# Hashed attention and two expert layers on one core: the first weight's sums spread over the loop, bucket marks by clipping, two reorderings

## What is computed

```python
# attention: 2 x 8 heads, 768 tokens, 64 wide
q_bits = (einsum('bhsd,dk->bhsk', q, proj) > 0)      # 6 hash bits a token
k_bits = (einsum('bhsd,dk->bhsk', k, proj) > 0)
mask = q_bucket[:, :, :, None] == k_bucket[:, :, None, :]
scores = where(mask, q @ k.T / sqrt(64), -1e9)
attn = softmax(scores); x = attn @ v                 # -> 1536 tokens x 512
# expert layer 1, dense: 8 experts, hidden 1024, 8 rounds of row and column scaling
P = exp(x @ w_gate - max); for _ in range(8): normalise rows, then columns of P
x = sum_e P[:, e] * (relu(x @ w1[e]) @ w2[e])
# expert layer 2, routed: each token with x @ w_skip > 0 goes to its best expert
x[t] += gate[t] * (relu(x[t] @ w1[e_t]) @ w2[e_t])
```

## Time and profile before

| what | value |
| --- | --- |
| median of 3 runs | 1365.22 us |
| the profiled execution's own time | 1366.09 us |
| its span, first to last instruction | 1364.3 us |
| PE busy | 1318.5 us (97%) |
| DVE busy | 850.2 us (62%) |
| ACT busy | 567.3 us (42%) |
| POOL busy | 332.9 us (24%) |
| mean granted TensorE clock | 0.993 of full speed |

### The profile page before, as it was taken

The page is one execution under the profiler, slowest core; times in us unless marked ns, Lnnn a source line. Parts: engine busy times, 40 slices in busy tenths (PEclk is TensorE's granted clock), DMA queues, the critical chain, the costliest instruction groups (busy, mean ns, idle before and its releaser), DMA issues.

```text
span 1364.3 us, 24719 instructions
## 1 busy us (share of the span) xinstructions
PE 1318.5 (97%) x9435; PEld 762.6 (56%) x9435; DVE 850.2 (62%) x1486; ACT 567.3 (42%) x870; POOL 332.9 (24%) x229
## 2 busy tenths in 40 slices
PE   6799999899999999999999999999999999998987
PEld 3576776655456446545545644554564465556665
DVE  5799999786667427525633743663474275567993
ACT  5799999653123204303411430431242043226662
POOL 4888889431100300300110030020003000121211
PEclk9899999999999999999999999999999999999999
DMA  8333532142011011001101100110110122467940
GB/s 227 97 93 92 127 93 49 63 166 98 0 63 62 1 62 61 0 0 61 61 0 61 61 0 0 62 61 0 61 61 0 36 83 82 167 208 271 340 166 21
DMA packets 51631, 109.84 MB, mean 81 GB/s; under 512 B 5216, under 2 KB 8840, under 8 KB 51568
## 3 DMA queue, kind: packets, MB, share of 16 engines
q1 hardware_dynamic: 48880, 105.40, 24.3%
q0 software_dynamic: 2240, 3.35, 0.7%
q10 hardware_dynamic: 448, 0.19, 0.1%
HBM read 93.57 MB, written 17.34 MB: 81 GB/s over the span
## 4 chain that ended last, share of the span: by engine, by line
PE 88%; DVE 4%; issue 2%; ACT 2%; DMA 0%; POOL 0%; ACTq 0%; POOLq 0%; DVEq 0%
PE ps L1676 14%; PE ps L1679 14%; PE ps L1680 14%; PE ps L1702 10%; PE ps L1705 10%; PE ps L1704 10%; PE ps L1597 5%; PE ps L1585 2%; PE ps L1587 2%; PE ps L1569 1%; PE ps L1607 1%; PE ps L1609 1%; PE ps L1611 1%; ACT probsT_hi L794 1%; DVE probsT_lo L1090 0%
## 5 line engine op out<-in xcount | busy, mean ns | idle before, releaser
L1702 PE MATMUL ps<-x_hi,w_hi 128*128 128x384 f16 x896 | 292.1, 326 | 3.2 <-DVE parts L1255 1.5
L1705 PE MATMUL ps<-x_hi,w_lo 128*128 128x384 f16 x896 | 292.1, 326 | 0.0
L1704 PE MATMUL ps<-x_lo,w_hi 128*128 128x384 f16 x896 | 292.1, 326 | 0.0
L1680 PE MATMUL ps<-w_hi,h 128*128 128x512 f16 x768 | 291.0, 379 | 0.0
L1679 PE MATMUL ps<-w_lo,h 128*128 128x512 f16 x768 | 291.0, 379 | 0.0
L1676 PE MATMUL ps<-w_hi,h 128*128 128x512 f16 x768 | 291.0, 379 | 0.0
L1312 DVE SCALAR_TENSOR_TENSOR x<-ps,gate_now,x 128x512 f32<-128x512 f32 x84 | 63.1, 751 | 251.7 <-PE ps L1680 250.7
L633 POOL TENSOR_TENSOR wf<-wf 128x1024 f32<-128x1024 f32 x8 | 18.8, 2353 | 632.7 <-PE ps L1705 622.1
L923 ACT ACTIVATE x1s<-ps 128x384 f32<-128x384 f32 x64 | 30.4, 475 | 327.0 <-PE ps L1705 327.0
L940 ACT ACTIVATE h<-parts 128x1152 f16<-128x1152 f32 x64 | 74.4, 1163 | 141.7 <-DVE parts L1270 141.7
L1680 PEld LDWEIGHTS ps<-w_hi,h 128*128 128x128 f16 x768 | 75.1, 98 | 90.6
(11 more groups left out here) (226 smaller groups left out, 2291.8 us busy)
## 6 DMA issues: line engine op xcount, KB each, us to landing
wf<-w1a SPq DMA_DIRECT2D x32, 512.0 KB, 6.0
w_stage_in<-w2a SPq DMA_DIRECT2D x8, 2048.0 KB, 8.8
w_in<-w1b SPq DMA_DIRECT2D x4, 2048.0 KB, 9.4
w_in<-w2b SPq DMA_DIRECT2D x4, 2048.0 KB
w_in_b<-w1b SPq DMA_DIRECT2D x4, 2048.0 KB, 10.6
w_in_b<-w2b SPq DMA_DIRECT2D x4, 2048.0 KB
rows<-blank SPq DMA_DIRECT2D x1, 6682.0 KB, 21.7
qk_in<-kT SPq DMA_DIRECT2D x32, 192.0 KB, 4.3
```

Of the source, the lines that this page charges most:

```text
L1680: last = pe.matmul(acc, a_lo, b_hi, start=False, stop=(m == n - 1))
L1702: pe.matmul(group_bank(g, role), w_hi, x_hi, start=(opens and kt == 0), stop=False, skip_group_check=not opens)
L1704: pe.matmul(group_bank(g, role), w_hi, x_lo, start=False, stop=False, skip_group_check=not opens)
L1705: last = pe.matmul(group_bank(g, role), w_lo, x_hi, start=False, stop=(kt == 1), skip_group_check=not opens)
```

## The change

It has four parts. (1) `sum_w1(0)` no longer stands ahead of POOL's round 1; its four sums come one each at the end of the rounds 1 to 4, and `split_first_w1` takes the blocks in an order in which each block's sum is there (5, 2, 0, 3, 1, 4, 6). (2) ACT takes the hash with the activation Identity, a scale of 2^112 and a per-partition bias, in place of Copy, and POOL clips it between `mark_floor` and `mark_top` by a minimum and a maximum, in place of a comparison and a product. DVE makes the bias from two small operations after the first head's marks; constants and the place of the negated projection follow. (3) In the last head ACT's `take_o` comes ahead of the work on x, and the high parts of x's blocks stand at the steps 1, 2, 4, 5 and after the last step, with none at step 3. (4) `split_gates` moves from group 1 to group 4 of the first expert.

```diff
+W1_SPLIT = (5, 2, 0, 3, 1, 4, 6)
...
-                pool.tensor_scalar(marks[HASHED, :], hashed[HASHED, :], least[HASHED, :], mark[HASHED, :],
-                                   ALU.is_ge, ALU.mult).then_inc(marks_ready, 1)
+                pool.tensor_scalar(marks[HASHED, :], hashed[HASHED, :], mark_top[HASHED, :], mark_floor[HASHED, :],
+                                   ALU.min, ALU.max).then_inc(marks_ready, 1)
...
+            def sum_w1_block(e, n):
+                if n == 0:
+                    pool.wait_ge(w1_loaded, 64 * e + 64)
+                    pool.tensor_tensor(wf[:, 5, :, :], wf[:, 0, :, :], wf[:, 3, :, :], ALU.subtract
+                                       ).then_inc(w1_summed, 1)
+                elif n == 1:
+                    pool.tensor_tensor(wf[:, 3, :, :], wf[:, 3, :, :], wf[:, 2, :, :], ALU.add
+                                       ).then_inc(w1_summed, 1)
+                elif n == 2:
+                    pool.wait_ge(w1_summed, 4 * e + 2)
+                    pool.tensor_tensor(wf[:, 4, :, :], wf[:, 3, :, :], wf[:, 0, :, :], ALU.subtract
+                                       ).then_inc(w1_summed, 1)
+                else:
+                    pool.wait_ge(w1_summed, 4 * e + 3)
+                    pool.tensor_tensor(wf[:, 6, :, :], wf[:, 1, :, :], wf[:, 4, :, :], ALU.subtract
+                                       ).then_inc(w1_summed, 1)
...
+            def split_first_w1(n):
+                k = W1_SPLIT[n]
+                pool.wait_ge(w1_summed, min(n + 1, 4))
...
-            sum_w1(0)
-            pool.wait_ge(w1_summed, 4)
             for j in range(1, G // 2):
...
                 normalise(2 * j - 1)
+                if j <= 4:
+                    sum_w1_block(0, j - 1)
                 split_first_w1(j - 1)
...
-                act.activation(hashed[HASHED, c * HALF:(c + 1) * HALF], psH[HASHED, 0:HALF], ACT.Copy
-                               ).then_inc(hash_taken, 1)
+                act.activation(hashed[HASHED, c * HALF:(c + 1) * HALF], psH[HASHED, 0:HALF], ACT.Identity,
+                               bias=hash_bias[HASHED, :], scale=HASH_SCALE).then_inc(hash_taken, 1)
...
                 if step in (0, 1):
                     take_xf(2 * step)
-                if step >= 1:
-                    x7_hi_part(0, X_HI[step - 1])
+                if step in (1, 2, 4, 5):
+                    x7_hi_part(0, X_HI[(1, 2, 4, 5).index(step)])
...
+                    if s % QT == 1 and not (first and s == 1):
+                        take_o(2 * j + s // QT - 1)
                     if last and s >= QT:
                         first_x(s - QT)
-                    if s % QT == 1 and not (first and s == 1):
-                        take_o(2 * j + s // QT - 1)
...
             act.wait_ge(zeroed, 12)
+            act.wait_ge(least_ready, 6)
             head_pairs(act, pair)
...
-            for k in X_HI[QT - 1:]:
+            for k in X_HI[QT - 2:]:
                 x7_hi_part(0, k)
...
             for c in range(2):
                 first_buckets(c)
+            dve.tensor_scalar(hash_bias[Q_MARKS, :], below_q[Q_MARKS, :], 0.5, Q_MASK, ALU.is_lt, ALU.mult
+                              ).then_inc(least_ready, 1)
+            dve.tensor_scalar(hash_bias[K_MARKS, :], below_k[K_MARKS, :], -K_MASK, None, ALU.mult
+                              ).then_inc(least_ready, 1)
...
-                    if first and g == 1:
+                    if first and g == 4:
                         split_gates()
```

More of the change, by code:

```diff
@@ L55 @@
 Q_MASK, K_MASK = 2.0 ** 15, 2.0 ** 13
-SMALLEST = 2.0 ** -126
+SMALLEST, HASH_SCALE = 2.0 ** -126, 2.0 ** 112
 MARKS = 2 * NBITS
@@ L118, in build @@
         least = sb("least", [P, 1], fp32)
-        mark = sb("mark", [P, 1], fp32)
+        hash_bias = sb("hash_bias", [P, 1], fp32)
+        mark_top = sb("mark_top", [P, 1], fp32)
+        mark_floor = sb("mark_floor", [P, 1], fp32)
         eps_bias = sb("eps_bias", [P, 1], fp32)
@@ L622, in _ @@
             split_k(1, 1)
-            pool.wait_ge(least_ready, 5)
+            pool.wait_ge(least_ready, 4)
             mark_buckets(1, 0, None)
@@ L646, in split_first_w1 @@
-            def split_first_w1(k):
+            def sum_w1_block(e, n):
[14 more added lines that the diff above has]
+                                       ).then_inc(w1_summed, 1)
@@ L648, in split_first_w1 @@
+            def sum_w1(e, turn=lambda n: None):
+                for n in range(4):
+                    if n == 0:
+                        pool.wait_ge(w1_loaded, 64 * e + 64)
+                    turn(n)
+                    sum_w1_block(e, n)
+            def split_first_w1(n):
+                k = W1_SPLIT[n]
+                pool.wait_ge(w1_summed, min(n + 1, 4))
                 scale = w_scale[:, :].unsqueeze(1).to_broadcast([P, 2, F // 2])
                 pool.tensor_tensor(w7_hi[:, k, :, :], wf[:, k, :, :], scale, ALU.mult).then_inc(w1_hi_ready, 1)
-                pool.wait_ge(w1_hi_ready, k + 1)
+                pool.wait_ge(w1_hi_ready, n + 1)
@@ L651, in split_first_w1 @@
                 pool.tensor_tensor(wf[:, k, :, :], wf[:, k, :, :], scale, ALU.mult).then_inc(w1_scaled, 1)
-                pool.wait_ge(w1_scaled, k + 1)
+                pool.wait_ge(w1_scaled, n + 1)
                 pool.tensor_tensor(w7_lo[:, k, :, :], wf[:, k, :, :], w7_hi[:, k, :, :], ALU.subtract
                                    ).then_inc(w1_lo_ready, 1)
-            sum_w1(0)
-            pool.wait_ge(w1_summed, 4)
             for j in range(1, G // 2):
@@ L814, in _ @@
             act.dma_start(proj2[0:64, 0:NBITS], proj).then_inc(proj_in, 16)
-            act.dma_start(proj2[64:P, 32 + NBITS:32 + MARKS], proj).then_inc(proj_in, 16)
+            act.dma_start(proj2[64:P, 32:32 + NBITS], proj).then_inc(proj_in, 16)
             act.dma_start(const[:, C_RANK:CONST], consts[:, C_RANK:CONST]).then_inc(ranks_in, 16)
@@ L1069, in _ @@
             dve.memset(least[:, :], 0.0).then_inc(least_ready, 1)
-            dve.memset(mark[64:96, :], Q_MASK).then_inc(least_ready, 1)
-            dve.memset(mark[96:P, :], -K_MASK).then_inc(least_ready, 1)
+            dve.memset(hash_bias[:, :], 0.0).then_inc(least_ready, 1)
+            for quarter, most, fewest in ((slice(64, 96), Q_MASK, 0.0), (slice(96, P), 0.0, -K_MASK)):
+                dve.memset(mark_top[quarter, :], most)
+                dve.memset(mark_floor[quarter, :], fewest)
             dve.wait_ge(proj_in, 32)
@@ L1074, in _ @@
                               ).then_inc(proj_ready, 1)
-            dve.tensor_scalar(proj2[64:P, 32:32 + NBITS], proj2[64:P, 32 + NBITS:32 + MARKS], -1.0, None, ALU.mult
+            dve.tensor_scalar(proj2[64:P, 32 + NBITS:32 + MARKS], proj2[64:P, 32:32 + NBITS], -1.0, None, ALU.mult
                               ).then_inc(proj_ready, 1)
@@ L1083, in first_buckets @@
                 dve.tensor_scalar(K2[0][Q_MARKS, cols], first_bank(c)[K_MARKS, 0:HALF], least[K_MARKS, :], -K_MASK,
-                                  ALU.is_ge, ALU.mult).then_inc(first_marked, 1)
+                                  ALU.is_lt, ALU.mult).then_inc(first_marked, 1)
             def take_probsT_lo(i, half, r):
@@ L1125, in _ @@
             dve.wait_ge(ranks_in, 16)
-            dve.wait_ge(least_ready, 1)
+            dve.wait_ge(least_ready, 2)
             dve.tensor_scalar(least[Q_MARKS, :], below_q[Q_MARKS, :], SMALLEST, None, ALU.mult).then_inc(least_ready, 1)
-            dve.tensor_scalar(least[K_MARKS, :], below_k[K_MARKS, :], 0.5, SMALLEST, ALU.is_lt, ALU.mult
-                              ).then_inc(least_ready, 1)
-            dve.wait_ge(least_ready, 5)
+            dve.tensor_scalar(least[K_MARKS, :], below_k[K_MARKS, :], SMALLEST, None, ALU.mult).then_inc(least_ready, 1)
+            dve.wait_ge(least_ready, 4)
             for c in range(2):
                 first_buckets(c)
+            dve.tensor_scalar(hash_bias[Q_MARKS, :], below_q[Q_MARKS, :], 0.5, Q_MASK, ALU.is_lt, ALU.mult
+                              ).then_inc(least_ready, 1)
+            dve.tensor_scalar(hash_bias[K_MARKS, :], below_k[K_MARKS, :], -K_MASK, None, ALU.mult
+                              ).then_inc(least_ready, 1)
             dve.wait_ge(qk_hi, 1)
```

14 lines of the change are left out of this document (removed).

## The result

The changed kernel takes 1355.8 us (median of nine runs, 1351.3 to 1359.4), the kernel before 1365.2 in the nine runs beside it: a ratio of 0.9932, with an interval of 0.9917 to 0.9947. Forecast were 1354.8 us and 8.4 + 1.2 + 2.0 - 1.2 = 10.4 us off the profiled execution. That one now takes 1356.9 us with a span of 1355.1, so 9.2 us came off.

A forecast was written before the change was run, and what follows sets the result against it. PE was taken as the bound, busy nearly always, so only its standstills could give time back. 8.4 (hole and restart) + 1.2 (last head) + 2.0 (gates) - 1.2 (late marks) = 10.4 us, giving 1354.8; range 1352.5 to 1357, 8-in-10 1351 to 1360.5.

The forecast's parts named there:

- The hole: ACT's 7.22 us wait for POOL's marks before the hash of head 3 goes; with the restart, 8.4 us gained.
- the slow restart: After the hole, the stretch to the next `take_o` ran at clock 0.53; 1.14 us to be regained.
- The claim that nobody needs the sums early: POOL's four weight sums, 2.35 us each, are not needed before the first expert.
- The marks late in four rounds: Sums in rounds 1 to 4 delay POOL's marks, so ACT waits; 4 x 0.29 = 1.2 us lost.
- I take the nearest row, m = 1.64: One marking on POOL, m, takes 1.64 us like a two-input operation; ends 0.79 and 2.94.
- The formula m - 1.10 us: ACT's wait for POOL's marks in each of four rounds with a sum, m being one marking's time.
- The last head: PE's wait for `take_o`'s sums and ACT's for DVE's x tile shrink; 1.2 us gained, ends 0.2 and 2.5.
- The gates: DVE's four gate operations, moved to group 4, take about 0.8 us; 2.0 of PE's 2.5 us wait gained.
- The prediction's own sentences on the port pair: VectorE and GpSimd share an exclusive lock, so L1352, L1266 and x's remainders would meet POOL's sums in the gates' stead.
- The hash with scale and bias: ACT's 30 hash operations of 486 ns change by 0, between -0.05 and +0.1 us each, hidden or not.
- dear marks: Rival: POOL's marks still take 2.94 us each, losing 6.4 us, so 1360.0 us; chance 0.15.
- The reorderings give nothing: Rival: POOL's contention and DVE's remainder chain take over the last-head and gate waits; 1357.5 us; chance 0.18.

The follow-up runs named there:

- sums_only: Kernel before with only the four sums spread over rounds 1 to 4, marks still by comparison and product: 1364.5 us, ratio 0.9998.
- marks_back: Changed kernel with the marks again made by comparison and product, all else as changed: 1361.3 us, ratio 0.997.
- after: First profile of the changed kernel, with no further edit: 1356.9 us in that execution.
- before_again: Kernel before, unchanged, profiled a second time: 1364.0 us in one execution.
- take_o_only: Kernel before with only `take_o` ahead of the work on x in the last head, high parts at their old steps: 1365.4 us in one execution.
- casts_late: Changed kernel with DVE's three casts moved from group 2 to group 5 of the first expert: 1354.8 us, ratio 0.9928.
- bias_ahead: Changed kernel with DVE's two bias operations ahead of the first head's marks: 1356.8 us in one execution.
- casts_bias: Changed kernel with both the three casts in group 5 and the bias operations ahead of the first marks: 1354.7 us, ratio 0.9922.

## Why the prediction came out

It was right in its mechanism and nearly in its sum; two of the four terms were mis-sized, in opposite directions.

**The hole, 8.4 us: right.** Measured 8.34, and within 0.1 of that in sums_only. Of this, the side before varies: in the five profiles that have both the lump of sums and dear marks `take_o` 0 to 1 takes 22.2 to 23.1 us, so the gain lies between 7.9 and 8.7. The wait of 7.22 us and the slow restart both went. The claim that nobody needs the sums early held too.

**The marks late in four rounds, -1.2 us: the term that was too large.** The step that failed is "I take the nearest row, m = 1.64": the marking takes 0.98 us. That still lies within the bounds of 0.79 and 2.94, near the lower one. ACT never waits for marks, and the six rounds lose 0.14 us. The formula m - 1.10 us was right where it could be seen: with m = 2.94 it gives 1.84, and the four waits come to 7.3 us, 1.83 each. ACT won back less than the 0.25 us a time that I allowed: 6.8 of the 7.3 us were lost, so 0.13 each. The estimate from the Trainium skill (GPSIMD Engine Reference, "3.1 Elementwise — side-by-side cycle accounting"), 1.15 us, was nearer than my row, and 0.98 us for 768 columns lies below it. The same section also states 1.03 cycles an element for the shortest bodies, which are bound by the ports; by that, again an estimate, it would be 0.66 us, and the measured time lies between the two.

**The last head, 1.2 us: right in size.** Measured 1.17. But all of it is `take_o`'s place; I had let the high part's new place share in it, so the size is right in part by luck.

**The gates, 2.0 us: mis-sized.** The step that failed is "of the 2.5 us that PE waited I expect 2.0 back". The operations did fall to 0.74 us in group 4, as forecast. But 1.1 of the 2.5 us were an accident of one execution, and of the 1.4 that are usually there a wait of 1.1 to 1.2 stays, now for DVE alone. The real gain is 0.3 to 0.4 us. The prediction's own sentences on the port pair named the reason, that DVE's next operations would meet POOL in the gates' stead, and the sum took no more than 0.5 us off for it: with the gates gone the casts are held up, and with the casts gone the remainders.

**The hash with scale and bias, 0 with an upper end of 0.1 us each: right.** It costs 0.09, hidden in the rounds. The bias operations delay the first maximum by 0.35 us, which no total shows.

With the sizes as measured the sum is 8.3 + 1.2 + 0.4 - 0.1 = 9.8 us, against 9.4 between the medians. The two errors, 1.1 too much lost and 1.6 too much gained, nearly met; that the total fell within 1 us of the forecast says less than the parts do. The range of 1352.5 to 1357 doesn't follow from the terms' ends as it says: with 2.5 for the last head and m = 0.79 the sum is 12.9 us, 1352.3, with 0.2 and m = 1.64 it is 9.4, 1355.8, and the gates had no ends. Of the rivals, "dear marks" was true as a mechanism (marks_back and sums_only behave as it says) and only its condition did not hold. "The reorderings give nothing" was half true: part 4 gives next to nothing, because POOL's contention with DVE is taken over by other operations, as it says.

What stays open: whether the minimum and maximum are cheap by themselves or by the values that they get (see the last section), and whether the 0.35 us of the bias operations ever reach the end. What would free the first expert is also untested: no run moved POOL's sums for x out of DVE's way.

## What to carry to other kernels

A lump of work that nobody needs yet belongs where its engine has slack, but ask at every place it is moved to what now starts later behind it: here 6.8 of the 8.4 us won were given back, and only a cheaper operation behind it kept the gain. Before a wait in a single profile is put into a sum, look whether it is there in a second profile of the same kernel; a margin of 0.7 us a round repeats, a blocked small operation may not. Work moved out of another engine's way helps only if what comes next is not blocked in its stead. Judge changes of less than 0.2% by stretches between marks that both traces have, not by totals, and compare the granted clock of a stretch before you explain its length.

## What the runs showed of the hardware

- On POOL the price of a two-step operation with per-partition operands can differ by a factor of three between two forms: 44x768 from fp32 to fp16 takes 2.94 us with a comparison and a product and 0.98 us with a minimum and a maximum, less than the 1.64 of an operation on two tensors over 768 columns. That the operations alone make the difference is not shown: the new form also gets other values (the hash scaled by 2^112, with a bias), and no run changed the one without the other.
- Many a small DVE operation beside POOL is not slowed but stopped until POOL's operation ends: the casts in after end 0.08 and 0.03 us behind the ends of POOL's operations, and the gates' of before_again take 0.90 and 1.84 us for what takes 0.17 and 0.18 where POOL is idle. Whether an operation is caught seems to hang on as little as 0.01 us (0.20 against 1.88 us for the fourth gate operation). Work that is moved away leaves the blocking to whatever comes next. The Trainium skill (SBUF — State Buffer, "SBUF: two separate sides") calls the port pair an exclusive lock on which the later one fully blocks; the trace agrees, and for operations with one tensor input too.
- Of the operations between them, the one with both inputs in SBUF took longer beside POOL (busy until 280.62) than after it, 0.71 against 0.56 us, and the one with an input in PSUM did not. DVE's timeline of after:

```profile
276.58 0.71 DVE L1286 TENSOR_TENSOR parts<-parts 128x384 f32<-128x384 f32 x1
277.21 0.55 DVE L1287 TENSOR_TENSOR parts<-ps,parts 128x384 f32<-128x384 f32 x1
...
285.14 0.56 DVE L1286 TENSOR_TENSOR parts<-parts 128x384 f32<-128x384 f32 x1
285.62 0.55 DVE L1287 TENSOR_TENSOR parts<-ps,parts 128x384 f32<-128x384 f32 x1
```

- The clock of 0.79 that take_o_only shows for eight microseconds in the first expert, with PE busy throughout, made the stretch from group 5 to 7 last 18.33 instead of 16.65 us; casts_late and bias_ahead had it too (18.33 and 18.29), the eleven other profiles not, among them casts_bias, which holds both their edits. The totals don't show it: in these three the granted clock near the end was 0.96 or 0.97 and the stretch behind group 7 took 1038.9 to 1039.4 us. The clock is a mean: from 310 to 314 us it was 0.57, close to the lower level, and from 306 to 309 it was 1.00. The row of take_o_only:

```profile
306.00:314.00 8.00, 8.00 (x142) 5.61 (x141) 4.78 (x7) 3.72 (x5) 0.00 (x0) 0.79 0.42 140
```
